# Attention, Fourier mixing and two MLPs in one kernel: the first batch's folds put inside a pair of score tiles, its transform pieces moved from slot 37 to slot 35, three groups of later scores behind tile 35

## What is computed

```python
scores = scale * np.matmul(q, k.transpose(0, 1, 3, 2))
kth = np.partition(scores, -32, axis=-1)[..., -32:-31]
scores = np.where(scores >= kth, scores, -1e9)
attn = softmax(scores); x = heads_side_by_side(attn @ v)
u = x + np.real(np.fft.fft(np.fft.fft(x, axis=1), axis=2))
un = (u - mean(u)) / np.sqrt(var(u) + 1e-6)
u = u + np.maximum(un @ moe_w_ch1, 0) @ moe_w_ch2
un = (u - mean(u)) / np.sqrt(var(u) + 1e-6) * g_ln
out = u + np.maximum(un @ moe2_w_ch1, 0) @ moe2_w_ch2
```

## Time and profile before

| | us |
|---|---|
| median of 3 runs (1359.71 to 1363.4) | 1361.39 |
| the profiled execution, device time | 1362.1 |
| its span, first to last instruction | 1360.3 |
| PE busy | 1252.0 (92%) |
| DVE busy | 1101.4 (81%) |
| ACT busy | 798.4 (59%) |
| POOL busy | 356.6 (26%) |

### The profile page before, as it was taken

How to read it: one execution, slowest core, us unless ns; L and a number is a source line. 1 busy time by engine, 2 the same in 40 slices (tenths; PEclk the granted TensorE clock), 3 DMA queues, 4 the chain that set the end, 5 groups by cost and what they waited for, 6 DMA issues and landing times.

```text
span 1360.3 us, 22775 instructions
## 1 busy us (share of the span) xinstructions
PE 1252.0 (92%) x7944; PEld 1024.3 (75%) x7944; DVE 1101.4 (81%) x2196; ACT 798.4 (59%) x1586; POOL 356.6 (26%) x327
## 2 busy tenths in 40 slices
PE   5776778999999899999988999999989999999999
PEld 3444444787777778788876888887679999999997
DVE  7999999899999989999999779975484454646453
ACT  4777765578777646776665557664353434343442
POOL 2444430122232431223335123333030111212110
PEclk9989978999999899999999999999999999999999
DMA  7899993567757757777885577753244343333342
GB/s 249 321 338 340 327 325 145 186 223 252 244 194 259 236 189 251 267 259 241 263 285 197 168 231 238 259 195 129 80 153 142 123 148 117 128 115 127 119 148 85
DMA packets 118259, 282.21 MB, mean 207 GB/s; under 512 B 29825, under 2 KB 29826, under 8 KB 118146
## 3 DMA queue, kind: packets, MB, share of 16 engines
q1 hardware_dynamic: 106386, 233.55, 51.7%
q10 hardware_dynamic: 10368, 42.47, 8.3%
q0 software_dynamic: 1392, 4.73, 1.1%
HBM read 237.44 MB, written 42.73 MB: 206 GB/s over the span
## 4 chain that ended last, share of the span: by engine, by line
PE 57%; DVE 36%; issue 5%; ACT 1%; POOL 1%; DMA 1%; SPq 0%; ACTq 0%; DVEq 0%
PE Big L752 23%; DVE top L1140 15%; PE Big L735 15%; DVE wk L1146 14%; PE Sp L735 7%; DVE ex L1153 3%; PE Tp L684 3%; PE Sp L779 2%; PE Tp L706 2%; PE Sp L791 1%; DVE st L1232 1%; PE Tp L811 1%; PE Big L779 1%; PE Sp L642 1%; PE Big L791 0%
## 5 line engine op out<-in xcount | busy, mean ns | idle before, releaser
L752 PE MATMUL Big<-wr,hh 128*128 128x512 f32 x1152 | 361.4, 395 | 0.0
L735 PE MATMUL Big<-uh,wr 128*128 128x256 f32 (+1 forms) x1400 | 320.9, 319 | 7.1 <-ACT hh L990 6.8
L1140 DVE MAX8 top<-wk 128x8 f32<-128x576 f32 x432 | 304.3, 745 | 0.0
L735 PEld LDWEIGHTS Big<-uh,wr 128*128 128x128 f32 x1400 | 236.5, 191 | 26.3 <-issue 16.5
L752 PEld LDWEIGHTS Big<-wr,hh 128*128 128x128 f32 x1152 | 217.6, 189 | 41.1
L752 PE MATMUL Big<-wr,hl 128*128 128x512 f32 x576 | 238.7, 414 | 4.8 <-DVE wr L1285 4.6
L512 POOL TENSOR_TENSOR hl<-hf,hh 128x256 fp32r<-128x256 f32 (+1 forms) x126 | 108.5, 861 | 452.5 <-ACT hh L990 452.5
L735 PE MATMUL Big<-ul,wr 128*128 128x256 f32 (+1 forms) x700 | 218.6, 312 | 0.0
L1146 DVE MATCH_REPLACE8 wk<-top,wk 128x576 f32<-128x576 f32 x288 | 211.4, 741 | 0.0
L684 PE MATMUL Tp<-ident,ex 128*128 128x128 f32 x720 | 117.1, 289 | 47.2 <-DVE ex L1153 38.3
L927 ACT ACTIVATE pT<-Tp 128x640 f32<-128x640 f32 x144 | 101.1, 702 | 88.1 <-PE Tp L684 87.9
(11 more groups left out here) (136 smaller groups left out, 1832.1 us busy)
## 6 DMA issues: line engine op xcount, KB each, us to landing
wf<-in_weights SPq DMA_DIRECT2D x208, 512.0 KB, 3.6
wr<-w_low SPq DMA_DIRECT2D x252, 256.0 KB, 4.3
sc<-in_weights SPq DMA_DIRECT2D x48, 512.0 KB, 3.2
sc<-sc_ahead ACTq DMA_DIRECT2D x36, 576.0 KB, 5.6
w_low<-wr SPq DMA_DIRECT2D x32, 512.0 KB, 6.6
sc_ahead<-U ACTq DMA_DIRECT2D x18, 576.0 KB, 5.2
sc_ahead<-un ACTq DMA_DIRECT2D x9, 576.0 KB, 4.1
sc_ahead<-yb ACTq DMA_DIRECT2D x9, 576.0 KB, 6.5
```

Of the source, the lines that this page charges most:

```text
L735: last = nc.tensor.matmul(hidden(n), a[:, kd * P:(kd + 1) * P], x[:, kd, 0:P * SIZE[p]], start=(kd == 0 and j == 0), stop=(kd == KD - 1 an ...
L752: last = nc.tensor.matmul(Ac[:, j, :], a[:, n % 2, j * P:(j + 1) * P], w, start=(f == 0 and m == 0), stop=(f == KF - 1 and m == 2))
L1140: nc.vector.max(top[:, s % RING, r, :], src).then_inc(s_top, 1)
```

## The change

DVE's `normal_x(0)`, `pair_x(0)` and `fold_x(0)` move from behind pair 18 to the middle of pair 18, behind its second round. The seam moves from slot 37 to slot 35, while `FIRST` stays at slot 39. On PE the groups of later scores 33, 34 and 35 move from the ends of slots 34, 35 and 36 to the end of slot 35, ahead of the pieces. ACT copies and stores group 32 at the end of slot 33 (before: in slot 34), and groups 33, 34 and 35 at the end of slot 35 (before: in slots 35, 36 and 37). The exponentials of tiles 38 and 39 move from the seam's beginning to behind its third piece (i = 2).

```diff
--- before.py
+++ after.py
@@ -38,6 +38,7 @@
 WFS = 3
 AHEAD = NT
 ASIDE = 4
+LAST = AHEAD - 1
 KEPT = TILES - 2 * AHEAD
 SIDE = (B // 2) * NHP
 
@@ -46,7 +47,7 @@
 BURST = 7
 GROUPS = len(ORDER)
 NUNITS = GROUPS * KF
-SEAM = NT + 1
+SEAM = NT - 1
 FIRST = NT + 3
 SCORED = {4: FIRST + 1, 5: FIRST + 2}
 DOUBLE = (45, 52, 59, 66, 71, 82, 87, 96, 101, 105, 111, 121, 126, 132, 138)
@@ -89,6 +90,18 @@
     return [n for n in range(NUNITS) if slot_of(n) == s - 1][-1:]
 
 
+def made_at(s):
+
+    if s == LAST:
+        return [LAST - 2, LAST - 1, LAST]
+    return [s - 1] if 0 < s < LAST - 1 else []
+
+
+def taken_behind(s):
+
+    return {LAST - 2: [LAST - 3], LAST: [LAST - 2, LAST - 1, LAST]}.get(s, [])
+
+
 def turn_slot(t):
 
     p, j = TURNS[t]
@@ -140,7 +153,7 @@
 
     if ready_pair(p) >= PAIRS:
         return START[p] - 10
-    return SEAM + 1 if p == 0 else 2 * (ready_pair(p) - 1)
+    return START[0] - 1 if p == 0 else 2 * (ready_pair(p) - 1)
 
 
 def width(c):
@@ -831,7 +844,7 @@
                         pe.wait_ge(s_unT_sb, last_turn(s))
                     probs_T(s)
                     if s + RING < KEPT and s not in SCORED.values():
-                        if last_piece(s) > last_piece(s - 1) > 0 or last_piece(s) == PIECES and s == SEAM + 1:
+                        if last_piece(s) > last_piece(s - 1) > 0 or last_piece(s) == PIECES and s == NT + 2:
                             pe.wait_ge(s_pc_sb, last_piece(s))
                         scores(s + RING)
                 for n in second_at(s - 1):
@@ -857,8 +870,8 @@
                     values_back(s)
                 for n in second_at(s):
                     mlp1(n)
-                if 0 < s <= AHEAD:
-                    scores_ahead(s - 1)
+                for e in made_at(s):
+                    scores_ahead(e)
                 if s == SEAM:
                     pe.wait_ge(s_tab, 48)
                     for b, i in pieces:
@@ -1043,7 +1056,7 @@
                     if s == START[0]:
                         for t in turns_at(s):
                             un_out(t)
-                    if 0 <= s - 2 < AHEAD:
+                    if 0 <= s - 2 < LAST - 3:
                         scores_aside(s - 2)
                     if s + RING < KEPT:
                         if s not in SCORED.values():
@@ -1093,11 +1106,15 @@
                             normalise(p, j)
                 if s % 2 == 1 and s + 1 < 2 * KF:
                     weights_high(s + 1)
+                for e in taken_behind(s):
+                    scores_aside(e)
+                    store_aside(e)
                 if s == SEAM:
-                    exps(s + 1)
-                    exps(s + 2)
                     for b, i in pieces:
                         piece_out(b, i)
+                        if i == 2:
+                            exps(START[0] - 1)
+                            exps(START[0])
                         if i == 0:
                             high_1(0)
                         if i == 1:
@@ -1145,6 +1162,10 @@
                         src = sc[:, s % RING, :] if r == 0 else wk[:, a, :]
                         nc.vector.match_replace(out=wk[:, a, :], in_to_replace=top[:, s % RING, r, :], in_values=src,
                                                 imm_value=STRUCK).then_inc(s_struck, 1)
+                    if n == NT // 2 and r == 1:
+                        normal_x(0)
+                        pair_x(0)
+                        fold_x(0)
                 for a, s in enumerate(tiles):
                     dve.wait_ge(s_exp, s + 1)
                     dve.wait_ge(s_top, t0 + 2 * (ROUNDS - 1) + a + 1)
@@ -1295,10 +1316,6 @@
             dve.wait_ge(s_init, 2)
             for n in range(PAIRS):
                 pair(n)
-                if n == NT // 2:
-                    normal_x(0)
-                    pair_x(0)
-                    fold_x(0)
                 if n == NT // 2 + 1:
                     combined(0, 0)
                     combine(0, 1)
```

## The result

| | before | changed |
|---|---|---|
| median of 8 runs, us | 1361.47 (1358.48 to 1363.4) | 1370.45 (1363.38 to 1375.82) |
| ratio to before, 95% interval | | 1.0073 (1.0058 to 1.0088) |
| profiled execution, device time | 1362.1 | 1375.14 |
| its span | 1360.3 | 1373.4 |

The change makes the kernel 0.73% slower by the ratio, about 10 us (the two medians lie 9.0 apart). The forecast was 1364.4 with a range up to 1367.2. The runs also spread over 12 us now, against 5 before, and the profiled execution lies at the upper end of them. So its terms add up to 13 us, not to 10.

A forecast was written before the change was run, and what follows sets the result against it. Prediction took PE, busy 92% of the span, as the bound, everything moving with the first MLP unit's start: -4.96 + 5.13 + 0.6 + 2.2 = +3.0 us, giving 1364.4 us, range 1359.7 to 1367.2.

The forecast's parts named there:

- Term 5: PE at the pieces' start: clock falls in the 2.4 us gap before them; +2.2 us, between 0 and 3.4.
- Terms 1 and 2: DVE's folds end earlier, PE's three score groups finish before them, so the pieces start at 222.65, not 227.61: -4.96 us.
- Term 3: PE slots 36 and 37 now stand uncovered between the last piece and slot 38: +5.13 us, bounds 4.0 to 5.5.
- Term 4: ACT's exponentials between third and fourth piece copies make the fourth copy late: +0.6 us, between 0 and 1.6.
- The clock stays up: Rival: PE's clock does not fall ahead of the pieces; +0.8 us, 1362.2 us; chance 0.25.
- The slower rival: PE's clock falls already within the three score groups, delaying the pieces and slowing them; +5.1 us, 1366.5 us; chance 0.13.
- The faster rival: Slots 36 and 37 cost nothing behind the pieces, filling waits PE has anyway; -4.4 us, 1357.0 us; chance 0.06.
- The long stage as a block of 1108 us: From the first MLP unit to the end, work only shifts with that unit's start, keeping 1108 us within 2 us.

The follow-up runs named there:

- c1_lift: Changed kernel with 24 identity transposes on PE behind piece 0; 1369.01 us, ratio 1.0056 to the kernel before.
- a1_fill: Changed kernel with 8, 8 and 16 unread identity transposes behind the three groups of later scores, filling PE's gaps; 1361.77 us, ratio 1.0010.
- a3_pe_part: Changed kernel with DVE's scaling and folds put back behind pair 18, seam still in slot 35; 1373.35 us, ratio 1.0089.
- d1_wide_in: Changed kernel with 6 unread float32 matmuls of 256 columns behind piece 0; 1369.49 us, ratio 1.0064.
- c3_last_gap: Changed kernel with 16 identity transposes behind group 35 alone, filling only the gap right before the pieces; 1364.03 us, ratio 1.0024.
- c4_woven: Changed kernel with PE's gaps from slot 34 to the pieces filled, slots 36 and 37's transposition and scores put behind pieces 3 and 7; 1359.07 us, ratio 0.9983.
- a4_hold: Kernel before with five extra unused BN_STATS on DVE ahead of the folds, giving PE a gap before the pieces; 1366.87 us, ratio 1.0057.
- a2_dve_part: Kernel before with only DVE's scaling and folds moved to the middle of pair 18, seam still in slot 37; 1369.88 us, ratio 1.0070.
- c2_before_fill: Kernel before with 16 identity transposes behind group 34, in PE's gap ahead of tile 36's transposition; 1358.66 us, ratio 0.9987.
- d2_wide_gaps: Changed kernel with its three gaps filled by 2, 2 and 4 float32 matmuls of 256 columns; 1362.25 us, ratio 1.0011.

## Why the prediction was wrong

- **Term 5, the clock, is the step that failed.** Its mechanism was right: a gap ahead of the pieces, then 1.2 GHz on work that nothing covers (the fall came 1.3 us behind the gap, though, at 224.5). Its size was not. The forecast put it at 2.2 us with an upper end of 3.4, because the two low stretches in rows 6 lasted 3.4 and 6.9 us. In the profiled execution it lasted about 24 us and cost 10.99. Over all runs the fill of the gaps gives back 1.0073 - 1.0010, which is 0.63% or 8.6 us. The upper end was no bound: I took the longest stretch seen as the longest possible, while the work at risk was 18.46 us of pieces that may double. Why the stretch is that long stays open.
- **Terms 1 and 2** gave -4.96; measured -4.47. The last copy of tile 35 ended at 215.00 as before, not at 214.6, since PE ran slot 34 at the low clock (tile 34's transposes 1.19 us, its scores 1.33, against 0.74 and 0.76 before). In c1_lift slot 34 ran at the high clock, the last copy ended at 214.69, and the pieces started at 222.82, close to the forecast's 222.65. In the changed kernel's profiled execution DVE idled 1.63 us for the 1.3 forecast.
- **Term 3** gave +5.13; measured 5.05. This is the step that takes the gain away, as forecast: the early folds only swap places with two slots.
- **Term 4** gave +0.6; measured 0.4 at the high clock (a1_fill), nothing in the changed kernel, where the copies lie 3.8 us apart.
- **The rivals.** "The clock stays up" would be +0.8 by the forecast; a1_fill, where it was up over the pieces, measured 0.1%, 1.4 us: close, but its first unit came 2.6 us later and its stage behind was shorter, so the match is in part luck. By itself the clock does not stay up. The slower rival had the right sign and, at 1366.5, half of the size. Its place, the clock falling within the groups, is not seen in the changed kernel's profiled execution, where the groups took 1.24 us each, but it is in c1_lift (at 218.5), which is the same program up to there, and in a3_pe_part (at 217.4). In d1_wide_in and c3_last_gap it fell earlier still, ahead of the groups, a place that no rival had. In all four the low clock then lasted 13.7 to 20.5 us, not 6.9. The faster rival did not come: slots 36 and 37 cost their full time.
- **The long stage as a block of 1108 us.** It took 1109.8 us in the changed kernel, inside the forecast's margin of 2 us, but 1105.2 to 1106.0 in nine of the ten experiments. Single executions of one stage differ by more than terms 3 and 4 were argued over, so a sum of such terms is not good to a few tenths.
- The rule quoted from the Trainium skill ("TensorE: Matmul & The Clock Gate", "A second HAM failure mode: psum-queue depth-cycling") named the right danger: short idles of PE between groups, and a clock that goes back and forth. The trace of c1_lift agrees with it in part, where the clock fell at 218.5 behind two groups with 1.23 us between them. The largest loss lay elsewhere, on pieces without gaps.

## What to carry to other kernels

Before moving long float32 matmul work right behind a wait, ask what PE does in the wait, and price the case in which the whole block runs at half the clock, not the longest low stretch that the trace happens to show. Throwaway transposes in the wait took 8.6 us of loss and most of the scatter away here (2.9 us between the lowest and the highest run, against 12.4). They cost nothing only where they end before the wait does: in c4_woven they delayed the groups by 0.9 us. Moving a block ahead of others on an engine that is busy from then on gains only what the engine idled; count first what now stands behind the block.

## What the runs showed of the hardware that was not expected

PE's clock can stay low while PE is busy without a pause: 0.51 over 24 us with PE busy 23.47 (changed kernel), 0.50 over 23.8 with 23.27 (a4_hold). The Trainium skill says in "TensorE: Matmul & The Clock Gate", section 'Part 1: The HAM clock gate (the "warmup" mystery)', that activity releases the throttle; these rows show sustained matmuls that did not release it for over 20 us, and the measurement decides.

These are all stretches at the low clock between 204 us and the first MLP unit, one profiled execution of each kernel, read from granted clocks in steps of 0.25 us:

| kernel | low clock, us | pieces, us |
|---|---|---|
| before | 218.6 to 225.4 | 227.6 to 246.1 |
| changed | 207.4 to 210.8; 224.5 to 248.4 | 223.1 to 252.6 |
| a1_fill | 211.8 to 218.6 | 224.6 to 243.5 |
| a2_dve_part | 218.7 to 235.8 | 237.6 to 256.1 |
| a3_pe_part | 207.2 to 210.6; 217.4 to 234.5 | 227.0 to 249.5 |
| a4_hold | 217.9 to 224.7; 231.6 to 255.5 | 229.9 to 259.4 |
| c1_lift | 218.5 to 232.2; 242.4 to 245.8 | 222.8 to 250.4 |
| c2_before_fill | none | 226.9 to 245.4 |
| c3_last_gap | 207.0 to 227.4; 241.1 to 244.5 | 228.1 to 248.6 |
| c4_woven | none | 224.0 to 244.6 |
| d1_wide_in | 212.0 to 232.5 | 226.2 to 250.7 |
| d2_wide_gaps | 211.7 to 218.5 | 224.6 to 243.5 |

The fall can come after the gap is over, with PE at work again: 1.3 us behind it in the changed kernel, 1.6 in a4_hold, 1.5 and 2.1 in the second stretches of c1_lift and c3_last_gap, which follow a wait of 0.93 us. So the instructions that run when the clock falls need not be those to blame. The same program falls at other places in other executions: up to the first piece the changed kernel, c1_lift and d1_wide_in are one program, and the first falls that reach their groups or pieces are at 224.5, 218.5 and 212.0.

Which executions get the long stretch is left to chance as far as these runs tell; a4_hold gave 1366.3 to 1366.9 three times and 1374.4 twice. What keeps the clock down was not found: matmuls of a like kind were followed by the high clock in d1_wide_in, and in a3_pe_part the pieces alone were. It stays open.
